# POOL's order in a routed two-stage kernel: expert entries fetched one tile ahead, routing scatters in pairs, the share taken with SiLU

## The reference

```python
def _attn_ref(r, k, v, w, u):                # 4 x 8 heads, 768 steps, head size 48
    for t in range(S):
        cur = einsum('bhd,bhe->bhde', u[None] * kt, vt)
        y[:, :, t] = einsum('bhd,bhde->bhe', rt, state + cur)
        state = w[None, :, :, None] * state + einsum('bhd,bhe->bhde', kt, vt)

def _moe_ref(x, w_in, w_out):                # 3072 tokens, 384 -> 2048 -> 384
    h = x @ w_in
    return (h * (1.0 / (1.0 + np.exp(-h)))) @ w_out

def _moe2_ref(x, modality_id, w_gate, modality_bias, w1, w2):   # 8 experts, 384 -> 1024 -> 384
    logits = x @ w_gate + modality_bias[modality_id]
    e_idx = np.argmax(logits, axis=1)
    ... probs = softmax(logits); gate_w = probs[arange(N), e_idx]
    for e in range(E):
        mask = e_idx == e
        out[mask] = gate_w[mask, None] * (np.maximum(x[mask] @ w1[e], 0.0) @ w2[e])
```

## Time and profile before

| | us |
|---|---|
| median of 3 runs | 812.1 |
| lowest and highest | 811.2, 813.39 |
| the profiled execution, its time | 811.17 |
| the profiled execution, its span | 809.6 |
| PE, busy in the span | 751.1 (93%) |
| PEld, busy | 728.8 (90%) |
| DVE, busy | 513.1 (63%) |
| ACT, busy | 436.2 (54%) |
| POOL, busy | 223.1 (28%) |
| DMA engines, mean | 130 GB/s |

### The profile page before, as it was taken

The page is one execution under the profiler, slowest core; times in us unless marked ns, Lnnn a source line. Parts: engine busy times, 40 slices in busy tenths (PEclk is TensorE's granted clock), DMA queues, the critical chain, the costliest instruction groups (busy, mean ns, idle before and its releaser), DMA issues. The chain is left out here.

```text
span 809.6 us, 24931 instructions
## 1 busy us (share of the span) xinstructions
PE 751.1 (93%) x9894; PEld 728.8 (90%) x9894; DVE 513.1 (63%) x1349; ACT 436.2 (54%) x1087; POOL 223.1 (28%) x337
## 2 busy tenths in 40 slices
PE   3589999999999999999999999997999999999984
PEld 3488899999999999999999998996999999999984
DVE  7779765776577655855686656315865665566552
ACT  4576545645464546555555555435555655655542
POOL 4422222142215221522242212102324223233331
PEclk9999999999999999999999999998999999999998
DMA  8931222212222222221222210223477656656661
GB/s 318 370 141 65 82 85 69 95 41 94 73 94 74 92 75 93 73 81 62 84 71 93 74 57 2 77 120 117 166 198 255 231 205 224 233 201 207 222 206 65
DMA packets 24159, 104.94 MB, mean 130 GB/s; under 512 B 4411, under 2 KB 9800, under 8 KB 20482
## 3 DMA queue, kind: packets, MB, share of 16 engines
q1 hardware_dynamic: 19362, 93.34, 33.4%
q0 software_dynamic: 4704, 10.29, 4.0%
HBM read 93.90 MB, written 10.11 MB: 128 GB/s over the span
## 5 line engine op out<-in xcount | busy, mean ns | idle before, releaser
L630 ACT ACTIVATE g<-ps_h 128x256 f32<-128x256 f32 x192 | 73.6, 383 | 205.4 <-PE ps_h L1018 152.3
L1016 PE MATMUL ps_h<-x_hi,wi_hi 128*128 128x256 f32 x576 | 165.9, 288 | 8.6 <-DVE x_lo L801 7.7
L1018 PE MATMUL ps_h<-x_hi,wi_lo 128*128 128x256 f32 x576 | 163.4, 284 | 0.8 <-issue 0.8
L1017 PE MATMUL ps_h<-x_lo,wi_hi 128*128 128x256 f32 x576 | 163.4, 284 | 0.0
L1033 PE MATMUL ps_o<-wo_hi,g_hi 128*128 128x392 f32 x384 | 135.5, 353 | 3.5 <-DVE g_lo L834 3.0
L1034 PE MATMUL ps_o<-wo_lo,g_hi 128*128 128x392 f32 x384 | 130.9, 341 | 0.1
L1035 PE MATMUL ps_o<-wo_hi,g_lo 128*128 128x392 f32 x384 | 130.4, 340 | 0.0
L834 DVE TENSOR_TENSOR g_lo<-g,g_hi 128x256 fp32r<-128x256 f32 x192 | 84.6, 445 | 68.8 <-ACT g_hi L623 66.8
L1016 PEld LDWEIGHTS ps_h<-x_hi,wi_hi 128*128 128x128 f32 x576 | 109.5, 190 | 11.5 <-DVE x_lo L801 7.9
L505 POOL TENSOR_TENSOR store<-store,up_half 128x256 f32<-128x256 f32 x44 | 34.4, 782 | 286.1 <-PE ps_y L1003 284.7
L1018 PEld LDWEIGHTS ps_h<-x_hi,wi_lo 128*128 128x128 f32 x576 | 109.8, 191 | 0.4 <-issue 0.3
(11 more groups left out here) (202 smaller groups left out, 1548.6 us busy)
## 6 DMA issues: line engine op xcount, KB each, us to landing
store<-in_w SPq DMA_DIRECT2D x28, 1536.0 KB, 9.1
store<-in_quads SPq DMA_DIRECT2D x48, 704.0 KB, 4.4
x_rows<-rows SPq DMA_DIRECT2D x12, 384.0 KB, 3.1
woT_raw<-in_woT SPq DMA_DIRECT2D x4, 768.0 KB, 10.4
wi_raw<-in_wi SPq DMA_DIRECT2D x4, 768.0 KB, 10.7
wo_raw<-in_wo SPq DMA_DIRECT2D x4, 768.0 KB, 12.2
store<-x_rows,entries POOLq DMA_INDIRECT x26
out_rows<-y,entries_out POOLq DMA_INDIRECT x26
```

The lines of the kernel that those rows point to most:

```text
L630: S.activation(g[:, F % 2, :], ps_h[F % 2][:, 0:ETOK], ACT.Silu).then_inc(g_made, 1)
L1016: T.matmul(out, hi, x_hi[:, t % 2, c, :], start=(c == 0), stop=False)
L1017: T.matmul(out, hi, x_lo[:, t % 2, c, :], start=False, stop=False)
L1018: last = T.matmul(out, lo, x_hi[:, t % 2, c, :], start=False, stop=(c == KC - 1))
```

## The change

`entries_new` is a new buffer. The load of a tile's entries goes into it, and `take_entries` copies it into `entries` when that tile's turn comes; right behind the copy the load for one tile further on is issued, and only then the gather. The two small copies and the waits on the results and on the gather stand in functions of their own (`shift_entries`, `results_landed`), in a new order. The table has one entry more. In the front block each scatter of four DMAs is split in two pairs: the first stands between `multiply_rk` and `scale_ends` of u = 17, 25, 33, 41, the second at the same place of the unit after. Group 4 stays whole and waits until the values of unit 46 are done. The sigmoid is replaced by SiLU of the distance minus one, and the arithmetic around it is adapted: with b the distance and s = SiLU(b - 1), s / ((b - 1) - s) is exp(b - 1), and the sum is multiplied by e.

```diff
@@ route_choose, route_gate
-    V.tensor_tensor(z.below[:], z.biased[:], best, ALU.subtract).then_inc(below_made, 1)
+    V.scalar_tensor_tensor(out=z.below[:], in0=z.biased[:], scalar=-1.0, in1=best, op0=ALU.add, op1=ALU.subtract).then_inc(below_made, 1)
...
-    link(V.tensor_scalar(z.below[:], z.share[:], -1.0, 1.0, ALU.mult, ALU.add))
+    link(V.tensor_tensor(z.below[:], z.below[:], z.share[:], ALU.subtract))
...
-    link(V.tensor_scalar(z.total[:], z.total[:], 1e-9, None, ALU.add))
+    link(V.tensor_scalar(z.total[:], z.total[:], math.e, 1e-9, ALU.mult, ALU.add))
@@ front_block, POOL
-            def scatter(m):
+            def scatter(m, blocks):
...
-                for n in range(TB):
+                for n in blocks:
...
             for u in range(2, QUADS):
                 multiply_rk(u)
+                if u % 8 == 1 and u >= 17:
+                    scatter(u // 8 - 2, (0, 1))
+                if u % 8 == 2 and u >= 17:
+                    scatter(u // 8 - 2, (2, 3))
                 scale_ends(u)
                 if u == 4:
                     routing_constants()
-                if u % 8 == 7 and u >= 15:
-                    scatter(u // 8 - 1)
+            pool.wait_ge(y_done, QUADS - 1)
+            scatter(4, (0, 1, 2, 3))
@@ front_block and experts_block, ACT
-                    S.activation(z.share[:], z.below[:], ACT.Sigmoid).then_inc(share_made, 1)
+                    S.activation(z.share[:], z.below[:], ACT.Silu).then_inc(share_made, 1)
@@ experts_block
-        TABLE = z.ETILES + 2
+        TABLE = z.ETILES + 3
+        entries_new = sb("entries_new", [P, EB, 2], I32)
@@ experts_block, POOL
             def load_entries(tiles, j):
                 row = pool.value_load(tiles[0:1, bass.ds(j, 1), 1:2], min_val=0, max_val=z.LIST - ETOK)
-                pool.dma_start(entries[:], z.lists[bass.ds(row, ETOK), :].rearrange("(b p) x -> p b x", p=P)).then_inc(entries_in, 16)
+                pool.dma_start(entries_new[:], z.lists[bass.ds(row, ETOK), :].rearrange("(b p) x -> p b x", p=P)).then_inc(entries_in, 16)
+
+            def take_entries(j):
+                pool.wait_ge(entries_in, 16 * (j + 1))
+                pool.sem_inc(pool_passed, 1)
+                nc.gpsimd.tensor_copy(entries[:], entries_new[:]).then_inc(entries_taken, 1)
+                pool.wait_ge(entries_taken, j + 1)
+                pool.sem_inc(pool_passed, 1)
...
-            def tile(tiles, j, first):
-                if not first:
-                    pool.wait_ge(y_out, 16 * EB * j)
-                    pool.sem_inc(pool_passed, 1)
+            def shift_entries(j):
                 nc.gpsimd.tensor_copy(entries_out[:], entries_next[:]).then_inc(entries_kept, 1)
                 pool.wait_ge(entries_kept, j + 1)
-                pool.wait_ge(x_gathered, 16 * EB * (j + 1))
                 pool.sem_inc(pool_passed, 1)
                 nc.gpsimd.tensor_copy(entries_next[:], entries[:]).then_inc(entries_moved, 1)
                 pool.wait_ge(entries_moved, j + 1)
                 pool.sem_inc(pool_passed, 1)
-                if not first:
-                    pool.wait_ge(listed, 16 * TB)
-                load_entries(tiles, j + 2)
+                pool.wait_ge(x_gathered, 16 * EB * (j + 1))
+                pool.sem_inc(pool_passed, 1)
...
             tiles = tiles_with_tokens(pool)
-            tile(table, 1, False)
+            pool.wait_ge(listed, 16 * TB)
+            load_entries(table, 3)
+            results_landed(1)
+            shift_entries(1)
             with pool.Fori(2, z.ETILES) as j:
                 with pool.If(j < tiles):
-                    pool.wait_ge(entries_in, 16 * (j + 1))
+                    take_entries(j)
+                    load_entries(table, j + 2)
                     gather(j)
                     results_out(j - 1)
-                    tile(table, j, False)
+                    results_landed(j)
+                    shift_entries(j)
```

More of the change, by code:

```diff
@@ L11 @@
+import math
 from contextlib import ExitStack
@@ L1163, in experts_block @@
         entries_moved = sem("entries_moved")
+        entries_taken = sem("entries_taken")
         x_gathered = sem("x_gathered")
@@ L1213, in _ @@
         def _(pool):
-            row = pool.value_load(z.first_tiles[0:1, 1:2, 1:2], min_val=0, max_val=z.LIST - ETOK)
-            pool.dma_start(entries[:], z.lists[bass.ds(row, ETOK), :].rearrange("(b p) x -> p b x", p=P)).then_inc(entries_in, 16)
-            table_constants(nc, z, TABLE, 2, table_consts_made)
-            nc.gpsimd.memset(z.ones[:], 1.0).then_inc(consts_made, 1)
             def load_entries(tiles, j):
                 row = pool.value_load(tiles[0:1, bass.ds(j, 1), 1:2], min_val=0, max_val=z.LIST - ETOK)
-                pool.dma_start(entries[:], z.lists[bass.ds(row, ETOK), :].rearrange("(b p) x -> p b x", p=P)).then_inc(entries_in, 16)
+                pool.dma_start(entries_new[:], z.lists[bass.ds(row, ETOK), :].rearrange("(b p) x -> p b x", p=P)).then_inc(entries_in, 16)
[5 more added lines that the diff above has]
+                pool.sem_inc(pool_passed, 1)
             def gather(j):
@@ L1252, in results_out, with results_landed @@
                                                  in_=y[:, i, :], in_offset=None, bounds_check=z.N - 1, oob_is_err=False).then_inc(y_out, 16)
-            pool.wait_ge(entries_in, 16)
+            def results_landed(j):
+                pool.wait_ge(y_out, 16 * EB * j)
+                pool.sem_inc(pool_passed, 1)
+            load_entries(z.first_tiles, 1)
+            table_constants(nc, z, TABLE, 2, table_consts_made)
+            nc.gpsimd.memset(z.ones[:], 1.0).then_inc(consts_made, 1)
+            take_entries(0)
+            load_entries(z.first_tiles, 2)
             for i in range(2):
@@ L1258, in _ @@
             gather(0)
-            tile(z.first_tiles, 0, True)
-            pool.wait_ge(entries_in, 32)
+            shift_entries(0)
+            take_entries(1)
             gather(1)
@@ L1268, in _ @@
             tiles = tiles_with_tokens(pool)
-            tile(table, 1, False)
+            pool.wait_ge(listed, 16 * TB)
+            load_entries(table, 3)
+            results_landed(1)
+            shift_entries(1)
             with pool.Fori(2, z.ETILES) as j:
                 with pool.If(j < tiles):
-                    pool.wait_ge(entries_in, 16 * (j + 1))
+                    take_entries(j)
+                    load_entries(table, j + 2)
                     gather(j)
                     results_out(j - 1)
-                    tile(table, j, False)
+                    results_landed(j)
+                    shift_entries(j)
             results_out(tiles - 1)
             pool.wait_ge(entries_in, 16 * (tiles + 1))
-            pool.wait_ge(y_out, 16 * EB * tiles)
-            pool.sem_inc(pool_passed, 1)
+            results_landed(tiles)
         @block.vector
@@ L1369, in tile @@
                         act.wait_ge(below_made, 1)
-                        nc.scalar.activation(z.share[:], z.below[:], ACT.Sigmoid).then_inc(share_made, 1)
+                        nc.scalar.activation(z.share[:], z.below[:], ACT.Silu).then_inc(share_made, 1)
                 act.wait_ge(w1_in, 16 * (j + 1))
```

## The result

The changed kernel takes 802.0 us (median of 4 runs, 801.5 to 803.3); the kernel before, beside it on the same chip, takes 812.4 (4 runs). The ratio is 0.989, 95% interval 0.986 to 0.991: 10.3 us faster, where 7 were forecast. Its profiled execution took 802.3 us, with a span of 800.7.

A forecast was written before the change was run, and what follows sets the result against it. PE, busy for 93% of the span, was taken to bound the kernel. From 811.2 us, -6.7 + 3.2 - 3.2 + 0.1 = -6.6 gave 804.6; with half of a 0.9 us offset carried, 805.0 us, range 800.5 to 808.5.

The forecast's parts named there:

- the likeliest case: Whole kernel: the forecast of 805.0 us, with bounds 803.5 to 807 and chance 0.51.
- rival A: Expert block, tile 2 costs little: gather 0.5 to 1.0 us later, clock stays up, 0.36 us waits go; 801.6 us, chance 0.27.
- Part 1: Expert block, tiles 3 on: entries loaded a tile ahead remove later gather waits, restarts and a lower-clock stretch; -6.7 us.
- D: Expert block, slower: gather and results run beside the w1 load and delay it on eleven tiles; 819 us, chance 0.04.
- Part 2: Expert block, tile 2: entries not fetched ahead, gather issued later behind the following load; turn +1.7, lower clock +1.55, sum +3.2 us.
- the lower clock: Expert block, tile 2: PE at 1.2 GHz after its gather wait, added as 1.55 us, bounds 0 to 3.3.
- the 2.6 worked out: Expert block, tile 2: PE's predicted wait for the gather before the third turn, 2.6 us.
- Part 3: Front block: paired scatters remove POOL's catch-up, so PE's four 0.81 us waits for keys go; -3.2 us.
- the four waits of 0.36 us: Front block, tile ends: PE's waits for g_lo, left open between 1.4 us gained and 1.6 lost, taken as 0.
- that scatter too holds DVE up: Front block: a scatter delays DVE's work, read from L766 ending 0.44 us late; bound 4 x 0.4 = 1.6 us lost.
- Part 4: Both blocks: SiLU removes table loads, ACT gains 12.8 us, PE nothing; sum +0.1 us, bounds 0 to 0.3.
- that cover: Front block: g made ahead keeps PE from waiting near ACT's table loads; without it 2.6 us per group would show.

The follow-up runs named there:

- the first four experiments: Changed kernel with 32 unused bytes ahead of xe_hi, 802.7 us; kernel before with them, 805.6; changed kernel with tile 1's entries_out copy early, 801.5; also gather before load, 799.4.
- before with the pad: The kernel before with 32 unused bytes allocated ahead of xe_hi and nothing else changed: 805.6 us, ratio 1.0004 to the kernel before.

## Why the prediction was right, and where not

**The time** fell inside the range and near its lower side; the likeliest case missed by 3 us, and of the cases rival A came nearest, for another reason than its own. That it came so close is partly luck: the sum had 5.0 us too little gain in the front block and nothing for the 2.5 us that the addresses cost, and the two misses have opposite signs.

**Part 1** (-6.7) held: 6.8 us of waits, restarts and clock went from the ten turns, and POOL waits for x and y there, not for entries. D's beginning did not show: a w1 or w2 load lands in 6.1 us at the median where it took 9.1.

**Part 2** (+3.2) had the right size (+3.5 at the third turn) and, in the changed kernel, the wrong wait; the lower clock came with it. The step that failed is the sentence that behind the moved issue stands `results_out(1)`, for which nobody waits soon. It counted DMAs and skipped the copy into `entries_out`, which ACT reads for `y`; that copy had stood ahead of the wait on `listed` and now stands behind it. With the copy early, the wait for the gather is 2.55 us against the 2.6 worked out, and the loss is the 3.2 us of the sum, yet without the lower clock that I had added: there the next turn was 1.3 longer at a clock of 1.00, because the results behind the late gather landed late and ACT stood 5.09 us for the copy behind them. So the same sentence on `results_out(1)` fails there too, and the agreement with 3.2 is in part chance (0.4 of it is the addresses).

**Part 3** (-3.2) was too small by 5.0 us, in two steps. First, the four waits of 0.36 us went as well, 4 x 0.4, since the reading that "that scatter too holds DVE up" was wrong: L771 takes 0.42 us inside a scatter. I had the earlier trace rows say it from one L766 of 0.87 us that ended 0.25 us behind the recorded start of POOL's next product; the rows beside scatters alone, all at 0.42 or 0.43, speak for that product as the neighbour that slowed it. Second, "the scatter of group 4 begins about 2 us later and stays 30 us ahead of the block's end" looked only at who waits for it, not at what it runs beside. (Within its tile it begins 0.9 us later, not 2.) In before its four scatters began beside PE's small products, and PE's own issue stopped again and again: 3.4 us at tile 10, which the later start took away. I had read PE's waits by releaser and passed over those that end with its own issue. The run with that wait alone and the pairs without it show this from both sides, on chips where the stall shows at all.

**Part 4** (+0.1): for PE SiLU is worth nothing, as forecast, but only because the scatters had been moved; by itself it costs 27 us. "If that cover were gone, 2.6 us per group would show" had the wrong sign and the wrong cover: what matters is not that the share comes late but that the places come early.

**Not in the sum at all:** the addresses, +0.2 us for each of 11 to 12 tiles, 2.5 us. The diff shows the line that moved them.

**Still open:** what stops PE's issue. On the chip of the first four experiments before with the pad has its scatter of group 4 at 496.48 us and the attention values at 496.67, as close as elsewhere, and no stall (tile 10: 40.00 us). The 804.5 us of before on that chip, against 811.5 to 812.4 on others, fits a kernel before that lacks the stall; no trace of before itself was taken there, and 3.4 us are only half of the difference. Code loading doesn't tell the kernels apart: the 16 KB instruction packet that starts 22.7 to 22.8 us into tile 10 takes 1.43 us in before and 0.94 in pairs alone, which stall, and 1.46 in the run with one wait and 0.95 in before with the pad, which don't. Nor is it known why the distance of operands matters, or why 160 is as good as 32 for one product and 128 worse for another.

## What to carry to other kernels

When a wait moves ahead on a queue, list every instruction behind it, the small copies too, and ask of each who reads what it writes. A step that becomes ready earlier can hurt: look at what it will then run beside, and pin it with a wait on that work, as one wait on `y_done` did here for 3.4 us. Where the kernel before is itself slow on some chips and not on others, a gain holds only for the chips on which it was measured. After adding any buffer compare the distance between the starts of the main matmuls with that of before, not their durations, and put small new buffers behind the operands of the inner loop.

## What the runs showed of the hardware that I had not expected

- Distances of operands: f32 matmuls of 256 columns start 0.1168 us apart with the two operands 32 bytes apart modulo 256, 0.1177 with 64, 0.1200 with 96, 0.1185 to 0.1187 with 128 (the front's `x_hi`, against 0.1169 with 32). With 384 columns it is 0.1734 at 32, 0.1755 to 0.1767 at 64, and 0.1735 at 96.
- Four indirect scatters of POOL (about 1 us each, 1.3 apart) that begin beside PE's products of 64x16 and 64x64 halve PE's issue, with 0.3 to 0.4 us of stall in each 0.73 us; in before another 1.6 us went in the dense 128x128 products behind, 0.84 of it in one wait. Scatters that begin beside dense products (159.65 us in before, 162.00 in after) show no such wait. Three kernels show it in their traces (before, pairs alone, SiLU alone) and one with the same order, on another chip, doesn't.
- A scatter of POOL leaves DVE operations of 128x256 with two inputs in SBUF at 0.42 to 0.43 us (19 in after); of those beside POOL's elementwise products some took 0.81 to 0.97.
